# A three-layer kernel whose last layer picks its first expert from half of the tokens' counts, lets GpSimd make one weight part and reads group numbers earlier

## What is computed

```python
x = attention(r, k, v, w, u)          # linear attention with decay: 4 x 768 tokens, 8 heads of 48
logits = x @ phi                      # soft mixture: 32 slots, 8 experts x 4 slots, w1 384x1024, w2 1024x384
slot_out[e] = relu((softmax_over_tokens(logits).T @ x)[e] @ w1[e]) @ w2[e]
x = softmax_over_slots(logits) @ slot_out
# routed mixture (moe2): each token goes to one of 8 experts
do = x @ w_skip > 0
e_idx = argmax(x @ w_gate, axis=1)    # among the tokens of do
for e in range(8):
    y[e_idx == e] = gate * (relu(x[e_idx == e] @ w1[e]) @ w2[e])
out = x + y                           # out = x for tokens that are not in do
```

## Time and profile before

| | us |
|---|---|
| median of three runs | 305.95 |
| lowest and highest run | 304.52 and 310.31 |
| the profiled execution's own time | 304.42 |
| its span in the profile | 302.7 |
| TensorE busy | 288.9 of 302.7 |
| VectorE, ScalarE, GpSimd busy | 182.2, 85.6, 64.7 |

### The profile page before, as it was taken

The page is one execution under the profiler, slowest core; times in us unless marked ns, Lnnn a source line. Parts: engine busy times, 40 slices in busy tenths (PEclk is TensorE's granted clock), DMA queues, the critical chain, the costliest instruction groups (busy, mean ns, idle before and its releaser), DMA issues.

```text
span 302.7 us, 8474 instructions
## 1 busy us (share of the span) xinstructions
PE 288.9 (95%) x3062; PEld 238.5 (79%) x3063; DVE 182.2 (60%) x422; ACT 85.6 (28%) x181; POOL 64.7 (21%) x103
## 2 busy tenths in 40 slices
PE   7899999999999999999898999999999999999993
PEld 7677788888878887643444878999989999899992
DVE  3699979888798897447542786352252622525232
ACT  1122222231322223503222865222213222122220
POOL 1489645455555320200000010000000000000000
PEclk9999999999999999999999999999999999999999
DMA  6999999887878979999999379802020020200202
GB/s 148 260 244 286 289 262 223 277 267 238 254 206 292 260 247 404 408 426 426 417 349 367 128 269 371 299 29 78 0 104 0 20 84 0 104 0 9 95 0 104
DMA packets 31311, 62.37 MB, mean 206 GB/s; under 512 B 4912, under 2 KB 22960, under 8 KB 30256
## 3 DMA queue, kind: packets, MB, share of 16 engines
q1 hardware_dynamic: 27824, 56.70, 56.8%
q10 hardware_dynamic: 3456, 5.25, 6.5%
HBM read 52.49 MB, written 9.44 MB: 205 GB/s over the span
## 4 chain that ended last, share of the span: by engine, by line
PE 89%; DVE 2%; SPq 2%; DMA 2%; issue 2%; ACT 1%; DVEq 0%; ACTq 0%
PE ps L1527 12%; PE ps L1528 11%; PE ps L1529 11%; PE ps L1257 8%; PE ps L1199 8%; PE ps L1280 4%; PE ps L1219 4%; PE ps L1538 4%; PE ps L1408 4%; PE ps L1427 4%; PE ps L1288 4%; PE ps L1269 3%; PE ps L1233 3%; DMA raw<-rT 2%; PE ps L1505 2%
## 5 line engine op out<-in xcount | busy, mean ns | idle before, releaser
L917 DVE SCALAR_TENSOR_TENSOR h_lo<-ps,h_hi 128x512 fp32r<-128x512 f32 x48 | 32.7, 690 | 65.2 <-ACT h_hi L1108 65.2
L1527 PE MATMUL ps<-w_hi,h_hi 128*128 128x384 f32 x192 | 65.5, 341 | 1.0 <-issue 0.5
L1528 PE MATMUL ps<-w_lo,h_hi 128*128 128x384 f32 x192 | 64.5, 336 | 0.0
L1529 PE MATMUL ps<-w_hi,h_lo 128*128 128x384 f32 x192 | 64.3, 335 | 0.0
L1108 ACT ACTIVATE h_hi<-ps 128x512 fp32r<-128x512 f32 x48 | 28.3, 599 | 80.6 <-PE ps L1538 74.5
L608 POOL TENSOR_TENSOR kt<-raw,dec_k 128x512 f32<-128x512 f32 x23 | 36.3, 1577 | 39.4 <-PE ps L1199 25.3
L1527 PEld LDWEIGHTS ps<-w_hi,h_hi 128*128 128x128 f32 x192 | 36.0, 188 | 5.3 <-issue 3.5
L1528 PEld LDWEIGHTS ps<-w_lo,h_hi 128*128 128x128 f32 x192 | 36.1, 188 | 1.3
L1529 PEld LDWEIGHTS ps<-w_hi,h_lo 128*128 128x128 f32 x192 | 36.1, 188 | 0.0
L738 DVE TENSOR_TENSOR at<-ps,mask 128x1024 f32<-128x1024 f32 x24 | 29.3, 1219 | 1.0 <-PE ps L1199 1.0
L1199 PE MATMUL ps<-rt,kt 48*128 48x128 f32 x384 | 27.9, 284 | 2.0 <-issue 0.8
(11 more groups left out here) (188 smaller groups left out, 371.3 us busy)
## 6 DMA issues: line engine op xcount, KB each, us to landing
w_first<-w1a SPq DMA_DIRECT2D x8, 768.0 KB, 7.0
w_first<-w2a SPq DMA_DIRECT2D x8, 768.0 KB, 8.2
a_slot<-w1a SPq DMA_DIRECT2D x4, 1536.0 KB, 14.7
x_slot<-w2a SPq DMA_DIRECT2D x3, 1536.0 KB, 13.2
out<-x SPq DMA_DIRECT2D x1, 4608.0 KB, 14.8
out<-x SPq DMA_DIRECT2D x24, 192.0 KB, 1.9
kn<-k_nat SPq DMA_DIRECT2D x20, 192.0 KB, 6.0
vn<-v_nat SPq DMA_DIRECT2D x20, 192.0 KB, 6.3
```

What stands on the lines that cost most here:

```text
L917: dve.scalar_tensor_tensor(out=h_lo[f % HB][:], in0=bank[4 + f % HB], scalar=0.0, in1=h_hi[f % HB][:].bitcast(F32), op0=ALU.max, op1=ALU.s ...
L1527: pe.matmul(bank[t][:, 0:DM], hh, w2_hi[:, f, :], start=(f == 0), stop=False)
L1528: pe.matmul(bank[t][:, 0:DM], hh, w2_lo[:, f, :], start=False, stop=False)
L1529: last = pe.matmul(bank[t][:, 0:DM], hl, w2_hi[:, f, :], start=False, stop=(f == FT - 1))
```

## The change

The first expert and its first group are found from the first half's counts alone. DVE does thirteen small steps on them (after.py L917 to L930) between the two halves of the routing, and PE's `count(1)` and outputs 12 to 15 move behind `slot_hidden(0)`. DVE copies the second half's counts to SBUF, and GpSimd and DVE build the table from there in turns. GpSimd also makes the first quarter of `w2_hi` (ACT did). Outputs 16 to 21 now stand behind `start_group` (before: 20 and 21). The exponentials of the gates move on ACT from behind output 10 into `rest_of_expert`. Filler matmuls (`keep_warm`) are added before and after the slots' outputs are turned, and the router's slot matmul is 120 columns wide instead of 10. `past_expert` is read late (`all_known`), and in `group` SP and DVE read the next group's numbers first instead of last. Tile 13 is taken by DVE too. The core of the diff:

```diff
@@ -50,10 +50,11 @@
     HB = 4
     AHEAD = HB - 1
     AHEAD_RAW = NRAW - 1
-    U_COUNT, U_FIRST, U_HIDDEN, U_QUARTER, U_EXP = 10, 16, 20, 22, 10
+    U_COUNT, U_HIDDEN, U_QUARTER = 12, 16, 22
     RL_REP, KEEP = 12, 8
     U_EARLY, RL_EARLY, RL_EVERY = 5, 10, 3
     RT = TILES // 2
+    HG = RT // GT
...
                 waits = [fixed(GT * ng + GT + t + 1) for t in range(GT)]
+                go_on(sp, g_at, more, e, g)
                 for t in range(GT):
                     sp.wait_ge(y_added, waits[t])
                     sp.dma_start(outv[:, bass.ds(g * GT + t, 1), :], x2[:, bass.ds(g * GT + t, 1), :]).then_inc(stored, 16)
-                go_on(sp, g_at, more, e, g)
 
             sp.wait_ge(first_known, 1)
...
+            steps = [0]
+
+            def settle(ins):
+
+                steps[0] += 1
+                ins.then_inc(table, 1)
+                pool.wait_ge(table, steps[0])
+
+            pool.wait_ge(first_known, 1)
+            e_first = load_first_expert(pool)
+            pool.wait_ge(w2q_in, 16 * FQ)
+            pool.tensor_copy(w2_hi[:, 0:FQ], w2_rows(e_first, 0)).then_inc(first_split, 1)
+
+            late = slice(HG, GROUPS)
+            pool.wait_ge(upto_set, 2)
+            pool.wait_ge(counts_ready, 1)
+            settle(pool.tensor_tensor(counts[:, :, 0:GT // 2], counts[:, :, 0:GT // 2], counts[:, :, GT // 2:GT], ALU.add))
+            settle(pool.tensor_tensor(pair_any[:, late], counts[:, :, 0], counts[:, :, 1], ALU.add))
+            settle(pool.tensor_scalar(pair_any[:, late], pair_any[:, late], 0.5, None, ALU.is_gt))
+            pool.tensor_tensor(pair_any[:, late], pair_any[:, late], bcast(upto[:, late], 2, E), ALU.mult).then_inc(pairs_ready, 1)
+            pool.wait_ge(nxt_ready, 1)
+            nxt_row = nxt[:].rearrange("p g e -> p (g e)")
+            settle(pool.tensor_scalar(exp_any[:], nxt[:, 0], 0.5, None, ALU.is_gt))
+            settle(pool.tensor_tensor(exp_any[:], exp_any[:], closed[:], ALU.mult))
+            pool.tensor_tensor(exp_index[:], exp_any[:], index[:], ALU.mult).then_inc(indexed, 1)
+            pool.tensor_scalar(exp_flag[:, 0:E], exp_any[:], 0.5, None, ALU.is_gt).then_inc(left_ready, 1)
+            settle(pool.tensor_scalar(left_flag[:], nxt_row, 0.5, None, ALU.is_gt))
+            settle(pool.tensor_scalar(nxt_row, nxt_row, -1.0, float(GROUPS), ALU.mult, ALU.add))
+            pool.tensor_scalar(next_group[:], nxt_row, float(GROUPS - 1), None, ALU.min).then_inc(left_ready, 1)
             pool.wait_ge(route_exp, 1)
             pool.tensor_tensor(rs4[:], ra[:, :, 0:E // 2], ra[:, :, E // 2:E], ALU.add).then_inc(gate_sum, 1)
             pool.wait_ge(gate_sum, 1)
...
                 dve.tensor_tensor(routed[:, tiles], rb[:, tiles], bcast(rc[:, tiles], 2, E), ALU.is_equal).then_inc(routed_ready, 1)
+
+            route(0)
+            dve.wait_ge(count_done, 1)
+            dve.wait_ge(upto_set, 1)
+            front = slice(0, HG)
+            link(dve.tensor_reduce(pair_any[:, front], bank[5][0:1, 0:RT * E].rearrange("p (g t e) -> p g e t", g=HG, t=GT), AX, ALU.max))
+            link(dve.scalar_tensor_tensor(out=pair_any[:, front], in0=pair_any[:, front], scalar=0.5, in1=bcast(upto[:, front], 2, E),
+                                          op0=ALU.is_gt, op1=ALU.mult))
+            link(dve.tensor_reduce(near[:], pair_any[:, front].rearrange("p g e -> p e g"), AX, ALU.max))
+            link(dve.scalar_tensor_tensor(out=exp_rank[:], in0=near[:], scalar=0.5, in1=rank[:], op0=ALU.is_gt, op1=ALU.mult))
+            link(dve.tensor_reduce(first_rank[:], exp_rank[:], AX, ALU.min))
+            dve.tensor_scalar(first_expert[:], first_rank[:], -1.0, float(E), ALU.min, ALU.add).then_inc(first_known, 1)
+            link(dve.tensor_scalar(first_rank[:], first_rank[:], -1.0, None, ALU.min))
+            link(dve.tensor_tensor(opened[:], rank[:], first_rank[:, 0:1].to_broadcast([1, E]), ALU.is_equal))
+            link(dve.tensor_tensor(near[:], near[:], opened[:], ALU.mult))
+            link(dve.tensor_reduce(last_near[:], near[:], AX, ALU.max))
+            dve.tensor_scalar(closed[:], opened[:], -1.0, 1.0, ALU.mult, ALU.add)
+            link(dve.tensor_scalar(last_near[:], last_near[:], float(GROUPS - HG + 1), -1.0, ALU.max, ALU.mult))
+            dve.tensor_scalar(first_group[:], last_near[:], float(GROUPS), None, ALU.add).then_inc(group_known, 1)
+            route(1)
             dve.sem_inc(w2lo_ready, WQ)
 
             def take_x2(u):
...
             dve.sem_inc(hlo_ready, HB)
             dve.sem_inc(y_added, GT)
 
-            def rest_of_expert(e, ne, ng):
+            def rest_of_expert(e, ne, ng, between=lambda: None):
                 low_of_g(1, ne)
+                between()
                 low_of_w2(1, e, ne)
                 low_of_g(2, ne)
                 low_of_w2(2, e, ne)
@@ -929,19 +965,34 @@
                 low_of_h(2, ng)
                 low_of_w2(3, e, ne)
 
+            e_first = load_first_expert(dve)
+            dve.wait_ge(count_done, 2)
+            dve.tensor_copy(counts[:].rearrange("p g t e -> p (g t e)"), bank[5][0:1, RT * E:2 * RT * E]).then_inc(counts_ready, 1)
+            low_of_g(0)
             take_x2(by_vector[0])
-            low_of_g(0)
-            take_x2(by_vector[1])
-            e_first = load_first_expert(dve)
+            dve.wait_ge(first_split, 1)
             low_of_w2(0, e_first)
             low_of_h(0, 0)
-            take_x2(by_vector[2])
+            take_x2(by_vector[1])
             low_of_h(1, 0)
-            take_x2(by_vector[3])
+            for u in by_vector[2:]:
+                take_x2(u)
+            dve.wait_ge(pairs_ready, 1)
+            for g in range(GROUPS):
+                last = dve.tensor_reduce(nxt[:, g], pair_any[:, g:GROUPS].rearrange("p g e -> p e g"), AX, ALU.max)
+            last.then_inc(nxt_ready, 1)
+            def last_expert():
+
+                dve.wait_ge(indexed, 1)
+                dve.tensor_reduce(last_index[:], exp_index[:], AX, ALU.max).then_inc(last_known_index, 1)
+                dve.wait_ge(last_known_index, 1)
+                dve.tensor_copy(past_expert[:], last_index[:]).then_inc(flags, 1)
+
+            g_at, more = loop_registers(dve)
+            rest_of_expert(e_first, 0, 0, last_expert)
             dve.wait_ge(gate_sum, 4)
             dve.reciprocal(rs1[:], rs1[:]).then_inc(gate_sum, 1)
...
+                        take_x2(u)
+
+            take_outputs(0, U_COUNT)
             act.wait_ge(first_known, 1)
             e_first = load_first_expert(act)
-            by_scalar_last = [u for u in range(U_FIRST, TILES) if by_scalar(u)]
+            act.sem_inc(w2hi_ready, 1)
             high_of_g(0)
-            take_x2(by_scalar_last[0])
-            act.wait_ge(w2q_in, 16 * FQ)
-            high_of_w2(0, e_first)
+            take_outputs(U_COUNT, U_HIDDEN)
             high_of_h(0, 0)
-            take_x2(by_scalar_last[1])
-            take_x2(by_scalar_last[2])
+            take_outputs(U_HIDDEN, U_HIDDEN + 1)
             high_of_h(1, 0)
-            for u in by_scalar_last[3:]:
-                take_x2(u)
-            past, g_at, more = loop_registers(act, e_first)
-            rest_of_expert(e_first, 0, 0)
+            take_outputs(U_HIDDEN + 1, TILES)
+            g_at, more = loop_registers(act)
+            def exps_of_routing():
+
+                act.wait_ge(route_shift, 2)
+                act.activation(ra[:], ra[:], ACT.Exp).then_inc(route_exp, 1)
+
...
             combine_by_slot(5, range(2))
+            keep_warm(2)
             out_by_channel(1)
             combine_by_slot(5, range(2, GT))
+            keep_warm(3)
             pe.wait_ge(sot_ready, E)
             pe.wait_ge(wr_in, 32)
             for k in range(KD):
-                last = pe.matmul(bank[2][:, 0:NR], so_t[:, k].rearrange("p r s -> p (r s)"), wr[:, k, :],
-                                 start=(k == 0), stop=(k == KD - 1))
+                last = pe.matmul(bank[2][:, 0:RL_REP * NR].rearrange("p (o r) -> p o r", r=NR), so_t[:, k].rearrange("p r s -> p (r s)"),
+                                 bcast(wr[:, k, :], 1, RL_REP), start=(k == 0), stop=(k == KD - 1))
             last.then_inc(sog_done, 1)
             for k in range(KD):
                 last = pe.transpose(bank[3][:, k * P:(k + 1) * P], so_t[:, k].rearrange("p r s -> p (r s)"), ident[:])
             last.then_inc(sog_done, 1)
+            keep_warm(1)
             pe.wait_ge(so4_ready, 1)
...
@@ -1495,9 +1552,6 @@
             count(0)
             for u in range(U_EARLY, U_COUNT):
                 first_output(u)
-            count(1)
-            for u in range(U_COUNT, U_FIRST):
-                first_output(u)
 
             def slot_hidden(q, e):
...
-            def rest_of_expert(e, ne, ng, start, free=None):
+            def rest_of_expert(e, ne, ng, start, free=None, ahead=lambda: None):
                 second(0, ng, ne, free)
                 pe.wait_ge(w1e_in[1], ne * 16 + 16)
```

(16 more changed lines are left out.)

102 lines of the change are left out of this document (42 added, 60 removed).

## The result

The changed kernel is slower by a little: the ratio of its time to that of the kernel before is 1.0088, 95% interval 1.0054 to 1.0121, with 22 runs of each. I had forecast 304.2 against 305.95, a ratio of 0.994.

A forecast was written before the change was run, and what follows sets the result against it. TensorE was taken as the bound (89% of the chain), SyncE's sequencer at the end. 304.42 + 0.66 (passage) - 1.2 (end) = 303.9, plus 0.3 excess for the median: 304.2 us; range 301.9 to 306.4.

The forecast's parts named there:

- Fillers (+0.25): Filler matmuls and 120-column slot matmul around the router's slot matmul: cost 0.25 us, bounds 0 and +0.9.
- First expert from half of the counts: In the routing: first_expert known at 171.3, 2.1 us earlier; slot_hidden(0) starts at 173.2, 1.87 earlier.
- second rival: In the second routing half, GpSimd's w2_hi copy holds up a VectorE product: 304.6 to 305.1; chance 18%.
- the lock: Exclusive port pair shared by VectorE and GpSimd, delaying routing and what follows by 0.7 to 1.2 us; chance 18%.
- Where the wait goes: Slot quarter to second(0): TensorE waits 1.25 and 0.75 us for outputs 15 and 17; passage ends 0.66 later.
- Read of past_expert covered: Before the third hidden row: TensorE's read done at 185.7, needed about 186; covered by 0.3 us.
- the two reads, 0, at most +0.5: VectorE's reads at the first group's head, some 1.4 us before the first h_lo: cost 0, at most +0.5.
- Table on GpSimd: Expert table built behind the routing: GpSimd's seven steps of about 0.35 us end near 184.8.
- The end: Last stores: SyncE's table reads leave the stretch before the span's end; gain 1.2 us, bounds 0.9 and 1.4.
- no stall: In the passage, DVE and ACT take outputs 15 and 17 before PE asks; second(0) 2.0 earlier, 301.9; chance 17%.
- another tail: At the end, SyncE's sequencer isn't what ends the kernel; the 1.2 gain is missing, 305.1; chance 7%.
- the table was late: Behind second(0), GpSimd's table is late: +0.5 to +1, giving 304.4 to 304.9; chance 8%.

The follow-up runs named there:

- e11: Changed kernel with the first high part of w2 made by ScalarE again, without GpSimd's copy: median 308.92 us, ratio 1.0108, six runs.
- e1: Changed kernel with VectorE's reads of left_flag and next_group put back behind the h_lo steps: median 306.09 us, ratio 1.0047.
- e16: Changed kernel again, unedited, as base of a later comparison: median 307.34 us, ratio 1.0027 to the kernel before.
- e3: Changed kernel with the 4608 KB store of x2 cut to its first tile: median 305.24 us, ratio 1.0003.
- e6: Changed kernel with 24 more register reads in a row behind GpSimd's last instruction: one execution, 305.84 us.
- e7: Changed kernel with VectorE's reads behind the h_lo steps and the 4608 KB store behind SyncE's read of past_expert: median 305.21 us, ratio 0.9979.
- e2: Changed kernel with VectorE taking outputs 15 and 17 a place earlier: median 307.85 us, ratio 1.0094.
- e5: Changed kernel with VectorE taking outputs 13, 15 and 17 ahead of w_lo and both h_lo: median 307.23 us, ratio 1.0016.
- e8: Changed kernel with outputs 13, 15, 17 taken early, VectorE's reads behind h_lo, and the store behind SyncE's past_expert read: median 304.06 us, ratio 0.9938.
- e14: The same kernel as e8 (changed kernel with three edits), in a second comparison: median 303.42 us, ratio 0.9927.
- e13: Changed kernel with five fillers ahead of output 19 and two ahead of output 21: median 307.06 us, ratio 1.0065, six runs.
- e12: Kernel before with the fillers, the wider slot matmul and SyncE's reads ahead of the stores: median 303.19 us, ratio 0.9904.
- e10: Kernel before with the fillers and the 120-column slot matmul alone: median 306.19 us, ratio 0.9983.

## Why the prediction was wrong, step by step

**Fillers (+0.25): wrong in sign.** The routing starts 0.19 earlier in the profile, and a mean clock under 0.988, which 72 of 114 executions of the kernel before have, is rare with fillers (6 of 166). I had the earlier trace rows with the idle 0.43 and saw a pause to be filled, not a place where the clock could fall, since it was 0.998 in the trace I read. The three runs on which I based the time (304.52, 305.95, 310.31) had the two levels in them; I called the difference an excess that nothing explains.

**First expert from half of the counts: right.** Known at 170.8 (forecast 171.3), slot quarter at 172.61 (173.2), distance from the routing 2.27 shorter (2.12 by my numbers). GpSimd's copy took 0.82 us (forecast 1.1) and ended at 172.59; VectorE's product with two SBUF inputs starts at 172.51 and takes 0.25 as before. So the second rival is out because the copy was short. The two overlap by 0.08 us alone, and the lock itself wasn't put to the test. e11 shows the copy to be worth its place.

**Where the wait goes: right as far as it went.** Slot to `second(0)` is 2.69 longer at full clock (8.11 against 5.42), forecast 2.53. (The split that I gave beside it, 1.87 won against 0.7 and 2.0, comes to a loss of 0.83 and not of 0.66; the 0.66 follows from the start times.) What the step lacks is what a pause can lead to: 1.65 more where the clock falls (9.76), 0.95 and 1.40 in e1 and e16. It fell in four of seven profiles with both pauses (after, e1, e11, e16; not e3, e6, e7) and in none of the five in which they were shortened, gone or filled (e2, e5, e8, e14, e13). That speaks for the pauses as its cause; why it falls in one run and not in the next isn't shown.

**"Read of past_expert covered" and "the two reads, 0, at most +0.5": the steps that failed.** I took 0.9 from the read's start to its use for one and 1.4 for the two, by reads outside the store, and moved them under a transfer that the kernel issues itself. Under it a read takes 0.86 to 1.03, and the two with what stands between them 3.0 (191.55 to 194.60). `past_expert` costs 0.74 (e3, e7: 0.1 to 0.2 when the read is short), and VectorE's two reads, ahead of `h_lo(3)`, 1.5 and as much again where the clock falls (e1: -2.9). "VectorE's sequencer runs ahead of its engine" was wrong at this place: the chain shows the sequencer's reads themselves as what `h_lo(3)` waited for, one behind the other. No row stood behind the 0.7 us that I gave TensorE in hand there. The Trainium skill has one figure here ("DMA: Bandwidth & Descriptors", section "Latency and other measured facts"): a floor of about 600 ns for a `tensor_load`. The traces don't agree: most reads take 263 to 320 ns, and under the store up to 1137.

**Table on GpSimd:** its last step ends at 186.1 (forecast 184.8), and TensorE reads at 186.3. Beside the read's length this is small: with short reads `second(0)` to `second(1)` is 0.13 (e3) and 0.22 (e7) above the kernel before's.

**The end: right.** -1.20 forecast and -1.20 measured; e12 against e10 gives -1.1 by itself.

**The sum.** Forecast at the profile's level -0.5, measured +4.5. The 5.0 between them are +1.65 and +1.6 for the two clock falls, +1.5 and +0.74 for the reads, -0.44 for the fillers and the start. The 1.7 us around the span, which I carried over, became 2.2, a further 0.5 that I had put at nothing. The range (301.9 to 306.4) had no case with a read or a clock in it. The clock falls aren't needed to leave it: four of the five executions of the changed kernel with a mean clock of 0.998 or more took 306.68 to 307.99, the fifth 306.38. The three executions behind my 305.95 were few as well; over 22 the kernel before's median is 308.29. Of the rivals, no stall, the lock and another tail didn't come; the table was late, at a price of 0.2 at most.

## What to carry to other kernels

Before you move a register read, look up what the DMA queues carry at its new place, and count each read that stands ahead of work for which another engine waits. Give a pause of TensorE two prices, its length and what it costs when the clock falls behind it: where the mean clock of some runs is 0.98 and of others 1.00, a few fillers can take microseconds off the median (2.5 here) though the best runs don't move. When a large change moves little, run its small parts alone: two of them together gave ratios of 0.990 and 0.994, the whole 1.009 and 1.003. Compare also what lies outside the spans.

## What I had not expected of the hardware

- A register read takes 0.26 to 0.32 us (an engine's first one 0.47 to 0.56), and 0.84 to 1.14 us while a store of 4608 KB runs at about 370 GB/s, on all five engines. Under the small last stores SyncE's took 0.52 and VectorE's 0.57. Reads under the loads of w1e and w2e alone weren't tried.
- TensorE's clock fell to 0.50 in an execution whose pauses ahead of it were 0.24 and 0.42 us, stayed down for about 10 us while TensorE was busy almost all the time, and cost 4.7 us. In other executions of the same code it held.
- Pauses of 1.13 and 0.45 us were followed by a fall in four of seven profiles, a wait of 1.7 to 1.8 us for `h_lo` in three of seven (after, e2, e5; not e6, e11, e13, e16). Once the pauses for the outputs were shortened or filled it fell behind them in no profile. In e8 and e14 it fell in the attention, behind pauses of 1.50 and 1.23 us that no other profile has.
